# A planner's table in a fused attention and two-layer expert kernel: the loads and block work of a unit placed some steps later

## The reference

```python
def _attn_ref(q, k, v, alpha):                 # B, H, S, D = 4, 8, 768, 48
    for t in range(S):
        state = alpha[:, :, t, :, None] * state + np.einsum('bhd,bhe->bhde', k[:, :, t], v[:, :, t])
        y[:, :, t] = np.einsum('bhd,bhde->bhe', q[:, :, t], state)

def _moe_ref(x, w_in, w_out):                  # 3072 tokens, 384 -> 2048 -> 384
    h = x @ w_in
    g = np.where(h > 0.0, h, alpha * (np.exp(np.minimum(h, 0.0)) - 1.0))    # alpha = 1
    return g @ w_out

def _moe2_ref(x, domain_probs, w1, w2):        # 4 experts, 384 -> 1024 -> 384
    p = domain_probs / (domain_probs.sum(-1, keepdims=True) + 1e-09)
    for e in range(E):
        out += p[:, e:e + 1] * (np.maximum(x @ w1[e], 0.0) @ w2[e])
```

## Time and profile before

| | |
|---|---|
| median of three runs | 1297.67 us |
| the profiled execution's own time | 1297.66 us |
| its span | 1295.9 us |
| PE busy | 1279.4 us (99%) |
| DVE, ACT, POOL busy | 851.4, 630.8, 505.2 us |
| granted TensorE clock, mean | 0.997 of full speed |
| DMA moved | 170.92 MB, mean 132 GB/s |

### The profile page before, as it was taken

The page is one execution under the profiler, slowest core; times in us unless marked ns, Lnnn a source line. Parts: engine busy times, 40 slices in busy tenths (PEclk is TensorE's granted clock), DMA queues, the critical chain, the costliest instruction groups (busy, mean ns, idle before and its releaser), DMA issues.

```text
span 1295.9 us, 24680 instructions
## 1 busy us (share of the span) xinstructions
PE 1279.4 (99%) x9681; PEld 1057.6 (82%) x9681; DVE 851.4 (66%) x1239; ACT 630.8 (49%) x1051; POOL 505.2 (39%) x416
## 2 busy tenths in 40 slices
PE   6999999999999999999999999999999999999999
PEld 6888888888888888888888888888888888888887
DVE  7797867666676765766676667676576645654445
ACT  3656444367534447634436743445763444653332
POOL 2671938512555731633852254672153300100011
PEclk9899999999999999999999999999999999999999
DMA  5436363264345236336335433524533333523320
GB/s 203 148 113 208 120 209 102 96 185 171 98 147 160 90 110 219 112 104 213 103 106 168 166 103 143 163 94 130 192 127 106 96 101 98 155 86 110 98 97 25
DMA packets 84343, 170.92 MB, mean 132 GB/s; under 512 B 29186, under 2 KB 30722, under 8 KB 84228
## 3 DMA queue, kind: packets, MB, share of 16 engines
q1 hardware_dynamic: 83936, 169.21, 40.2%
q10 hardware_dynamic: 292, 0.14, 0.0%
HBM read 163.24 MB, written 6.08 MB: 131 GB/s over the span
## 4 chain that ended last, share of the span: by engine, by line
PE 94%; DVE 3%; issue 1%; ACT 1%; DMA 0%; ACTq 0%; DVEq 0%
PE ps_o L674 15%; PE ps_h L674 15%; PE ps_h L676 15%; PE ps_h L675 15%; PE ps_o L676 14%; PE ps_o L675 14%; PE ps_att L652 1%; PE ps_att L610 1%; PE ps_att L579 1%; PE ps_att L499 1%; DVE w_lo L873 1%; PE ps_att L513 1%; DVE g_lo L889 0%; PE ps_att L560 0%; DVE k_level L809 0%
## 5 line engine op out<-in xcount | busy, mean ns | idle before, releaser
L873 DVE TENSOR_TENSOR w_lo<-w_stage,w_hi 128x768 fp32r<-128x768 f32 x288 | 333.2, 1158 | 26.6 <-ACT w_hi L1098 23.7
L674 PE MATMUL ps_o<-g_hi,w_lo 128*128 128x512 f32 x864 | 341.5, 395 | 0.3 <-DVE g_lo L889 0.2
L674 PE MATMUL ps_h<-x_hi,w_lo 128*128 128x512 f32 (+1 forms) x861 | 335.5, 390 | 1.6 <-DVE x_lo L913 1.6
L676 PE MATMUL ps_o<-g_hi,w_hi 128*128 128x512 f32 x864 | 336.6, 390 | 0.0
L675 PE MATMUL ps_o<-g_lo,w_hi 128*128 128x512 f32 x864 | 336.6, 390 | 0.0
L676 PE MATMUL ps_h<-x_hi,w_hi 128*128 128x512 f32 (+1 forms) x861 | 334.8, 389 | 0.0
L675 PE MATMUL ps_h<-x_lo,w_hi 128*128 128x512 f32 (+1 forms) x861 | 334.7, 389 | 0.0
L1129 ACT ACTIVATE g_hi<-ps_h 128x512 fp32r<-128x512 f32 x184 | 110.1, 598 | 443.3 <-PE ps_h L676 443.2
L893 DVE SCALAR_TENSOR_TENSOR g_lo<-ps_h,g_hi 128x512 fp32r<-128x512 f32 x184 | 126.9, 689 | 243.9 <-ACT g_hi L1129 243.9
L319 POOL TENSOR_TENSOR products<-blocks 128x384 f32<-128x384 f32 x150 | 201.1, 1356 | 157.6 <-DVE scores L792 109.8
L1098 ACT CAST w_hi<-w_stage 128x768 fp32r<-128x768 f32 x288 | 239.2, 832 | 14.5 <-DMA w_stage<-in_w 13.1
(11 more groups left out here) (115 smaller groups left out, 971.7 us busy)
## 6 DMA issues: line engine op xcount, KB each, us to landing
w_stage<-in_w SPq DMA_DIRECT2D x288, 384.0 KB, 3.0
k_level<-in_k SPq DMA_DIRECT2D x12, 512.0 KB, 5.8
q_low<-in_q SPq DMA_DIRECT2D x12, 512.0 KB, 6.6
alpha<-in_a SPq DMA_DIRECT2D x12, 512.0 KB, 4.3
v_tok<-in_v SPq DMA_DIRECT2D x12, 512.0 KB, 4.8
p_rows<-p_norm SPq DMA_DIRECT2D x6, 1024.0 KB, 8.5
values_states<-in_v_heads SPq DMA_DIRECT2D x20, 256.0 KB, 4.5
out<-acc SPq DMA_DIRECT2D x18, 256.0 KB, 3.9
```

The costliest lines, as they stand in the source:

```text
L674: nc.tensor.matmul(dst, lhs[1], rhs[0], start=first, stop=False)
L676: return nc.tensor.matmul(dst, lhs[0], rhs[0], start=False, stop=last)
L873: nc.vector.tensor_tensor(wl[n % WRING][:], stage[n % STAGE][:], wh[n % WRING][:].bitcast(F32), ALU.subtract).then_inc(w_low, 1)
```

## The change

The table of steps is changed. In tile 0 the loads of unit 2 move from ahead of step 0 to steps 2 and 8, and those of unit 3 from steps 8 and 11 to 14 and 22. Their low, block and place work goes later too. In the later tiles the loads of the odd unit move from steps 8 and 11 to 12 and 15, and its block work stays at step 18. The fourth `state` update of a unit goes one step later. At the layer change, `w_lo` of slice 18 is no longer made in step 14 but in step 15, behind `x2_lo`. Nothing is added or taken away.

```diff
-STATES_AT = {6: (0,), 7: (1, 2), 9: (3,)}
+STATES_AT = {6: (0,), 7: (1, 2), 10: (3,)}
...
 PARTS_AT = {
-    "unit": ((None, 8), (-STEPS + 26, 8)),
-    "blocks": ((None, 11), (-STEPS + 29, 11)),
+    "unit": ((2, 14), (-STEPS + 26, 12)),
+    "blocks": ((8, 22), (-STEPS + 29, 15)),
     "v": ((None, 2), (-STEPS + 30, 2)),
-    "low": ((0, 18), (-STEPS + 33, 18)),
-    "block": ((0, 18), (-STEPS + 35, 18)),
-    "place": ((13, 31), (-STEPS + 46, 31)),
+    "low": ((5, 20), (-STEPS + 33, 18)),
+    "block": ((10, 22), (-STEPS + 35, 18)),
+    "place": ((22, 35), (-STEPS + 46, 31)),
...
@@ SP, before step 0
-            load_unit(LEAD)
-            load_blocks(LEAD)
...
@@ DVE, step J
                 if j == N1 - 1:
                     lower_x2(t)
+                    lower_w(J + SPLIT - 1)
                     lower_relu(J + 1)
...
-                if J + SPLIT < ALL:
+                if J + SPLIT < ALL and j != N1 - AHEAD:
                     lower_w(J + SPLIT)
```

## The result

| | median, us | lowest to highest | runs |
|---|---|---|---|
| before, same chip | 1297.62 | 1296.75 to 1298.90 | 15 |
| changed | 1300.57 | 1298.92 to 1303.41 | 15 |

The ratio is 1.0024, with a 95% interval of 1.0017 to 1.0030: the changed kernel is slower by 2.95 us. The profiled execution took 1300.13 us (span 1298.3), 2.47 us more than that of before. The forecast was 1301.3.

What follows compares the result with a forecast made beforehand. PE, busy for 1279.4 us, was taken to bound the kernel, so only its waits or own work could move the time. Sum: 1297.66 - 2.2 (gains) + 5.8 (loss at step 22 of tile 0) = 1301.3 us, range 1299.3 to 1303.0.

Steps and rivals of the forecast that it cites:

- DVE's wait for POOL in front of it: Tile 0, step 24: DVE's reduce waits for POOL's first product of unit 3, itself waiting for block tensors landing at 166 to 168.
- the 1.93 us behind L650: Layer changes of tiles 1 to 4: PE's next matmul follows after 1.9 us (line called L652 before the change).
- the short one a step later: Sign in PE's list of waits: a short wait for DVE one step after `hidden(28)`, costed at 0.7 us.
- The wait in `hidden(28)`: Tile 0: PE starts at 170.8, 5.0 us late, behind late block tensors; sign: a 4 to 6 us wait at about 166.
- The second wait: Tile 0, `hidden(29)`: second product late, `w_lo(29)` and `g_lo(27)` end at 178.2, PE wants them at 177.0; taken as 0.7 us.
- The layer changes: Tiles 1 to 4: one `w_lo` and the state update leave `x2_lo`'s way, three waits go; gain 1.5 us.
- Tile 4's `g_lo(15)`: Less POOL work beside the ELU steps: PE's 0.23 us wait for a slow `g_lo` goes; gain 0.4 us with restart.
- Tile 0: Steps 1 to 9: unit 2's low and block work no longer fill them together, one gap goes; gain 0.3 us.
- The upper bound of 2.7 for the gain: Gain of 2.2 us bounded by 0 and 2.7 us, the latter with nothing new anywhere and a few small gaps gone.
- A: Tile 0, step 24: wait covered if tensors land some 5 us sooner or cover is larger; only gains stay, 1295.5 us; 22%.
- B: Delay goes on: POOL late with all of unit 3, PE waits 1 to 4 us more at the key update; 1304.3 us; 12%.
- C: Layer-change waits come from ACT's `x2_hi` or go over to `g_lo(15)`; gain 0.7 instead of 2.2, 1302.8 us; 10%.

Runs made afterwards that it cites:

- the order alone: Kernel before with only the layer-change order altered (`w_lo` split ahead of x2's low parts, last state a step later): 1296.42 us, ratio 0.9993.
- the loads alone: Kernel before with only the odd units' loads moved, to steps 12 and 15 from 8 and 11: 1295.71 us, ratio 0.9988.
- tile 0 as before: Changed kernel with tile 0's table entries and early loads of the kernel before: 1296.18 us, ratio 0.9988.
- the kernel with sooner block loads: Changed kernel with unit 3's three block tensors loaded at step 20 of tile 0 instead of 22: 1294.47 us, ratio 0.9974.

## Why the prediction was right

The verdict and the mechanism held: one wait for DVE in `hidden(28)` behind POOL and the block tensors, and the waits for `x2_lo` gone. The sum was 1.2 us too high against the profiled execution (+3.6 for +2.47), and of its terms several were off and cancelled, so that it came so near is partly luck. Of the signs named beforehand, the one wait in `hidden(28)`, DVE's wait for POOL in front of it and the 1.93 us behind L650 came; the block tensors landed at 164.9 us and not at 166 to 168, PE's wait was 3.9 us for 4 to 6, and the short one a step later was missing.

- *The wait in `hidden(28)`: 5.0 predicted, 4.04 measured.* The first block tensor went out at 159.07 for 160.2: SP began the step at 148.66 instead of 150.6, and the values held it for 1.94 us where the earlier trace rows have 1.18. The third landed after 4.9 us; I took the median of ten, 5.8. Product, reduce, `w_lo(28)` and `g_lo(26)` took 3.5 us from 165.14, 3.8 predicted. All that makes 2.1 us sooner; but PE was there 1.16 us sooner too, which I had not carried from the gains into this step.
- *The second wait: 0.7 predicted, none.* From the first product's end to the second's it took 6.1 us (166.13 to 172.22), not 7.7. And PE came late by itself, since its clock had fallen. `g_lo(27)` was ready at 174.80, `hidden(29)` wanted it at 176.6.
- *The clock behind the pause: not in the sum, 1.7 us measured.* This is the term that the prediction left out, and none of its rivals named it. That the loss came out at 5.76 us against 5.8 predicted is chance: 1.0 and 0.7 too much, 1.7 too little. The Trainium skill ("TensorE: Matmul & The Clock Gate", section "HAM oscillation — how this bites in real kernels") says that waits of TensorE between groups of matmuls can bring the clock down, and that the matmuls behind them then start at the lower one, a cost on top of the wait. The two traces with the longest pauses agree (0.55 over 3.8 us and 0.60 over 6.8 us behind them), and it was the rule to weigh beside a forecast wait of 5 us.
- *The layer changes: 1.5 predicted, 1.55 measured.* Right in size, but with one cause named where two were at work. The order of DVE's queue was said to free `x2_lo`; the later loads of the odd units do it as well, as the kernels with one of them show.
- *Tile 4's `g_lo(15)`: 0.4 predicted, 0.51 measured,* and only the loads bring it.
- *Tile 0: 0.3 predicted, 0.84 measured behind the start,* and 1.7 between medians (1296.18 and 1294.47). I counted the one gap that had a row of its own, 0.3 us, and it is 0.38 by the shifts. The others, of about 0.1 and 0.2 us, lie where DVE's and POOL's work lay together, and no list names them. The trace of before is also a mild one: in the traces of the order alone, the loads alone and tile 0 as before, which keep its tile 0, this stretch takes 0.23 to 0.60 us more than in it, and in all with the changed tile 0 it takes 0.84 to 0.87 less. The rest of the 1.7 may lie ahead of step 0, where the first hidden matmul came between 48.65 and 50.28 us in the twelve traces, early and late with either set of loads. The upper bound of 2.7 for the gain had allowed 0.5 for small gaps. With them, gains were 2.90 us in the trace and 0.32 up to the first hidden matmul, for 2.2 predicted.
- *Rivals.* A (the wait covered, 1295.5) is what the kernel with sooner block loads does, at 1294.5: with its condition met, the price was right to 1 us. B did not come: PE's list has no wait for the key update. C did not either: the waits at the layer changes of tiles 1 to 3 and that for tile 4's `g_lo(15)` went, and none took their place.

## What to carry to other kernels

A load that is moved to a later step also moves behind whatever that step has put in its queue; here 8 us of another unit's store, wait and loads stood there (151.07 to 159.07 us), and two steps earlier, or one place further up in the queue, turned a loss of 0.24% into a gain of 0.26%. Where two edits could each take away the same wait, run each alone before both are kept: here a table entry made a new order of instructions needless. A pause of TensorE has to be priced above its length: in the two traces with the longest ones 1.7 and 2.6 us came on top, for matmuls at the lower clock. One trace does not settle that price where it varies from execution to execution: with a pause of 3.1 us the traced execution was the fastest of 11 and 2.2 us below their median.

## What the runs showed of the hardware

- TensorE's granted clock fell at a pause in the middle of dense matmuls: it was 1.00 through a pause of 3.9 us, 0.55 in the 3.8 us behind it, and 1.00 again; in one of 4.1 us it fell while PE still stood (0.83 over the pause), and it was 0.60 in the 6.8 us behind. Behind pauses of 3.1 and 1.7 us it stayed at 1.00 in the executions profiled. A mean of 0.996 or less over a whole execution came in 12 of the 41 executions with one of these pauses and in none of 144 without.
- A `w_lo` of 128x768 took 0.96 us on VectorE with GpSimd idle (743.99 us, the loads alone) and 2.07 beside GpSimd's updates of `k_level` and the decays (745.03 us, before); a `g_lo` of an ELU step took 0.69 and up to 1.55.
- Two loads of 256 KB each held SP's queue for 1.94 us in one place and 1.18 us in another. A wait for a store on that queue, from the store's issue to the next issue, took 4.2 us (151.07 to 155.25), and all that stood behind it left later.
